# Seven products instead of eight in the first batch's last matrix product, with the folded weights split early and kept in DRAM

## What is computed

```python
def _moe_ref(x, domain_probs, w1, w2):          # x (1536, 512), w1 (4, 512, 1024), w2 (4, 1024, 512)
    p = domain_probs / (domain_probs.sum(-1, keepdims=True) + 1e-09)
    for e in range(E):
        h = np.maximum(x @ w1[e], 0.0)
        out += p[:, e:e + 1] * (h @ w2[e])

def _moe2_ref(x, w1, w2, w3, w_out):            # w1, w2 (512, 1024), w3 (1024, 1024), w_out (1024, 512)
    a = x @ w1
    b = x @ w2
    h = a * b @ w3
    return h @ w_out
```

## Time and profile before

| | |
|---|---|
| median of 3 runs | 793.29 us (792.9 to 794.73) |
| time of the profiled execution | 793.14 us |
| its span, first to last instruction | 791.3 us |
| mean granted TensorE clock | 0.998 |
| busy in the span: PE, POOL, DVE, ACT | 785.2, 537.3, 480.8, 340.1 us |
| gated layer of the first batch on PE | to 429.81 us |
| last product of the first batch on PE | 429.81 to 464.60 us |

### The profile page before, as it was taken

The page is one execution under the profiler, slowest core; times in us unless marked ns, Lnnn a source line. Parts: engine busy times, 40 slices in busy tenths (PEclk is TensorE's granted clock), DMA queues, the critical chain, the costliest instruction groups (busy, mean ns, idle before and its releaser), DMA issues.

```text
span 791.3 us, 14038 instructions
## 1 busy us (share of the span) xinstructions
PE 785.2 (99%) x4702; PEld 747.4 (94%) x4702; DVE 480.8 (61%) x1045; ACT 340.1 (43%) x731; POOL 537.3 (68%) x501
## 2 busy tenths in 40 slices
PE   9999999999999999999999999999999999999997
PEld 8777779999999999999999899999999999999997
DVE  6896687513533633624866438458568569688771
ACT  5576785432431521522444337317327327333341
POOL 3589898694683765658497427938938848944772
PEclk9999999999999999999999999999999999999999
DMA  7943565965564544636199723472472581568512
GB/s 249 401 167 113 196 223 199 369 237 196 200 238 155 213 173 186 219 150 237 72 342 378 286 65 116 126 270 104 145 274 81 154 288 64 155 204 307 182 27 85
DMA packets 53628, 155.19 MB, mean 196 GB/s; under 512 B 6176, under 2 KB 12336, under 8 KB 53552
## 3 DMA queue, kind: packets, MB, share of 16 engines
q1 hardware_dynamic: 50176, 147.24, 51.9%
q10 hardware_dynamic: 3312, 6.95, 2.5%
q0 software_dynamic: 64, 0.03, 0.1%
HBM read 103.31 MB, written 50.88 MB: 195 GB/s over the span
## 4 chain that ended last, share of the span: by engine, by line
PE 98%; POOL 1%; ACT 0%; DVE 0%; issue 0%; ACTq 0%
PE bank L50 30%; PE bank L52 30%; PE bank L51 30%; PE bank L627 3%; PE bank L637 3%; PE bank L656 3%; PE bank L243 1%; POOL pr L513 1%; PE bank L257 0%; ACT pr L520 0%; POOL bl L1354 0%; ACT pt L537 0%; DVE end L2387 0%; DVE rden L589 0%; DVE blank L2811 0%
## 5 line engine op out<-in xcount | busy, mean ns | idle before, releaser
L50 PE MATMUL bank<-bh,ah 128*128 128x384 f32 x672 | 225.3, 335 | 0.1
L52 PE MATMUL bank<-bh,al 128*128 128x384 f32 x672 | 224.6, 334 | 0.0
L51 PE MATMUL bank<-bl,ah 128*128 128x384 f32 x672 | 224.5, 334 | 0.0
L50 PEld LDWEIGHTS bank<-bh,ah 128*128 128x128 f32 x672 | 126.2, 188 | 1.4 <-issue 0.7
L51 PEld LDWEIGHTS bank<-bl,ah 128*128 128x128 f32 x672 | 126.2, 188 | 0.1
L52 PEld LDWEIGHTS bank<-bh,al 128*128 128x128 f32 x672 | 126.2, 188 | 0.0
L50 PE MATMUL bank<-sh,ah 128*128 128x384 f32 x280 | 93.8, 335 | 0.0
L52 PE MATMUL bank<-sh,al 128*128 128x384 f32 x280 | 93.6, 334 | 0.0
L51 PE MATMUL bank<-sl,ah 128*128 128x384 f32 x280 | 93.6, 334 | 0.0
L1295 POOL TENSOR_TENSOR al<-raw,ah 128x512 fp32r<-128x512 f32 (+1 forms) x60 | 71.9, 1215 | 26.7 <-ACT ah L1289 26.7
L50 PE MATMUL bank<-hh,w2h 128*128 128x384 f32 x256 | 85.5, 334 | 0.0
(11 more groups left out here) (183 smaller groups left out, 1628.1 us busy)
## 6 DMA issues: line engine op xcount, KB each, us to landing
raw<-weights SPq DMA_DIRECT2D x56, 512.0 KB, 3.5
splits<-ah SPq DMA_DIRECT2D x24, 896.0 KB, 4.1
splits<-al SPq DMA_DIRECT2D x24, 896.0 KB, 6.3
ah<-splits SPq DMA_DIRECT2D x48, 256.0 KB, 3.5
al<-splits SPq DMA_DIRECT2D x48, 256.0 KB, 4.3
ah<-splits SPq DMA_DIRECT2D x24, 384.0 KB, 4.7
al<-splits SPq DMA_DIRECT2D x24, 384.0 KB, 5.7
k<-k SPq DMA_DIRECT2D x8, 704.0 KB, 6.8
```

What stands on the lines that cost most here:

```text
L50: nc.tensor.matmul(out, wh, xh, start=start, stop=False, skip_group_check=adds_on)
L51: nc.tensor.matmul(out, wh, xl, start=False, stop=False, skip_group_check=adds_on)
L52: return nc.tensor.matmul(out, wl, xh, start=False, stop=stop, skip_group_check=adds_on)
```

## The change

The first batch's last product is made by channels with seven products too. For that the gated groups of the first batch make the sums T1 to T4 over pairs as the second batch does (`gated_group`, `pair_sum`), and DVE also takes the low parts of T1 and T2 (`pair_split_low`); POOL takes those of T3, T4 and B11 behind the weight splits. The folded weights come as four pieces `("fold", e)`, one in each expert of the first batch, are split like a group's weights, stored, and loaded for both batches (`load_last`); their splitting at the end of the second batch goes away. The raw slots and half of the gate tile serve as room for sums and outputs in between, so `down_sums` of the second batch's second down piece comes later. In both last products the second half (d = 1) has another order of products, `LAST_ORDER`. The output is by channels for both batches. The diff, cut to its core:

```diff
+LAST_ORDER = (1, 2, 6, 5, 7, 4, 3)
...
-            order += [("up", g + 4), ("up", g + 5), ("up", g + 6)]
+            order += [("fold", e), ("up", g + 4), ("up", g + 5), ("up", g + 6)]
         order += [("up", g) for g in range(19, UPS)]
-        order += [("last", j) for j in range(4)]
-        order += [("down", n) for n in range(2 * DOWNS * (E + 1))]
+        order += [("down", n) for n in range(2 * DOWNS * E)]
...
+    def stores(self, sp, t, d, *places):
+
+        for p, done in enumerate(((11, 22), (21,), (12,))):
+            for r in places:
+                self.load_split(sp, r, p)
+            for c in done:
+                self.store_end(sp, t, d, c)
...
         j += 1
+        if self.batch_of(stage) is not None:
+            self.down_group(pe, j, 1, (0, 1))
+            self.down_group(pe, j, 6, (0, 1))
+            self.down_group(pe, j, 1, (2, 3))
+            self.down_group(pe, j, 5, (0, 1))
+            self.down_group(pe, j, 2)
+            self.down_group(pe, j, 6, (2, 3))
+            self.down_group(pe, j, 5, (2, 3))
+            for p in (7, 4, 3):
+                self.down_group(pe, j, p)
+            return
...
-        pe.wait_ge(self.drained, 8 * E)
-        self.y_step(pe, t, 0, 0)
...
-        for r in range(3, ROWS_OUT):
-            for k in range(KF):
-                self.y_step(pe, t, r, k)
+        self.down_groups(pe, (E + 1) * t, i0 + KF - 1)
...
             if q == 1:
-                self.pair_high(act, p, T1)
-            self.gated_kept(act, q)
...
+                self.pair_high(act, t, p, T1)
+            self.gated_kept(act, t, q)
+            if t == 0 and q < KF - 3:
+                self.up_high(act, self.ring(i0 + q + 3))
             if q % 2 == 0:
                 if p:
-                    self.pair_high(act, p - 1, T3)
...
+                    self.pair_high(act, t, p - 1, T3)
+                    self.pair_high(act, t, p, T1)
+            elif q < KF - 1:
+                self.gated_h22(act, t, p)
+                self.pair_high(act, t, p, T2)
+                self.pair_high(act, t, p, T4)
...
         self.sums_low(pool, i0 + 1, T1, T2, T3)
+        if e == 0:
+            self.down_sums(pool, 1)
         self.parts_low(pool, e, 2, 5)
...
+    def first_gated_gpsimd(self, pool):
+
+        on, r = self.nc.gpsimd, self.ring(KH * E + 3)
+        self.up_sums(pool, r)
+        self.b_split_low(pool, on, B22, 1)
+        self.up_low(pool, r)
+        for n in range(1, KF - 3):
+            self.up_sums(pool, r + n)
+            self.up_low(pool, r + n)
+        for p in range(KH - 1):
+            self.gated_h11_low(pool, 0, p)
+        for p in range(KH):
+            self.pair_lows(pool, 0, p, T3)
+            if p == KH - 2:
+                self.gated_h11_low(pool, 0, p + 1)
+            self.pair_lows(pool, 0, p, T4)
+        for b in (B11, B21, T1, T2, B22):
+            self.b_split_low(pool, on, b, 2)
+        self.down_sums(pool, 0)
...
+    def pair_split_low(self, dve, p, b):
+
+        dve.wait_ge(self.t_high, self.pair_count(0, p, b))
+        self.nc.vector.tensor_tensor(self.sl[b][p][:, :], self.pair_raw(0, p, b), self.sh[b][p][:, :].bitcast(F32),
+                                     ALU.subtract).then_inc(self.t4_low, 1)
+
+    def gated_group(self, dve, t, q):
+        p = q // 2
 
         def rest():
             if q and q % 2 == 0:
-                self.pair_h_low(dve, p - 1, 22)
-                self.pair_sum(dve, p - 1, T3)
+                self.pair_h_low(dve, t, p - 1, 22)
+                self.pair_sum(dve, t, p - 1, T3)
             if q == 1:
-                self.pair_sum(dve, p, T1)
-            if q == KF - 1:
-                self.down_s1_s3(dve, self.nc.vector, 2 * DOWNS * E + 2)
-
-        self.gated_sums(dve, 1, q, rest)
+                self.pair_sum(dve, t, p, T1)
+            elif t == 0 and q % 2:
+                self.pair_split_low(dve, p, T1)
+
+        self.gated_sums(dve, t, q, rest)
         if q % 2 == 0:
             if q:
-                self.pair_sum(dve, p, T1)
+                self.pair_sum(dve, t, p, T1)
+            if t == 0 and q:
+                self.pair_split_low(dve, p - 1, T2)
             return
```

More of the change, by code:

```diff
@@ L993, in transfers @@
         kind, n = self.pieces()[m]
-        return 4 if kind == "down" and n >= 2 * DOWNS * E else 1
+        return 4 if kind == "fold" else 1
     def wait_raw(self, eng, kind, n):
@@ L1042, in gate_load @@
     def gate_load(self, eng, n):
+        if n == E:
+            for s in range(2):
+                eng.wait_ge(self.y_stored[s], 16 * (DOWNS * len(ENDS) // 2))
         if n > E:
@@ L1174, in up_quarters, with groups_before, wait_loaded @@
-    def up_quarters(self, g):
-        raw, s = self.raw_of("up", g), self.a_sum
+    def groups_before(stage):
+        if stage == 0:
+            return UPS - KH
+        return UPS + KH * (stage - 1) + (0 if stage <= E else KF - KH)
+    def wait_loaded(self, eng, r, a):
+        p = [a in part for part in LOADS].index(True)
+        s = self.slot_at(r)
+        nth = sum(self.slot_at(q) == s and self.user(q)[0] != "down" for q in range(RING0, r + 1))
+        eng.wait_ge(self.split_loaded[s][p], 32 * nth)
@@ L2187, in gpsimd @@
-        for j in range(4):
-            self.out_low(pool, "last", j)
-        for b in (B11, B21, B22):
-            self.b_split_low(pool, on, b, 2)
-        for n in range(2):
-            self.down_sums(pool, n)
+        self.first_gated_gpsimd(pool)
         for e in range(E):
```

813 lines of the change are left out of this document (399 added, 414 removed).

## The result

The changed kernel takes 801.8 us in the median of 6 runs (798.68 to 803.45), the one before 793.73 us beside it: 0.94% slower, ratio 1.0094 with a 95% interval of 1.0071 to 1.0117. The forecast was 799.5 us, range 795.0 to 802.0. The profiled execution is the slowest of the six, 803.45 us, span 801.4; it had 0.8 us more of stops while `Fold` ran than the kernel before, ahead of anything that was changed, so it is read here for its stops and not for its total. A stop is time in which PE starts no matmul; a step (k = 0 to 3) of a product of the last product is the three matmuls for one pair of groups, and a piece of the folded weights is one quarter of them, two steps of each product. A lock is DVE and POOL holding each other up.

The account below looks back on a forecast made before the run. The prediction took TensorE (PE), busy 99% of the span, as the bound, with POOL full in two stages. Its terms: 793.14 − 3.59 − 0.4 + 5.6 + 0.6 + 1.8 + 2.4 = 799.55, forecast 799.5 us, range 795.0 to 802.0.

Parts of the forecast that it names:

- Matmuls, −3.59: First batch's last product: 168 matmuls taking 29.12 us replace 32.71 us, saving 3.59 us.
- Splits at the end, −0.4: End of the second batch: PE's stalls from splitting the folded weights go away, saving 0.4 us.
- Gated layer, +5.6: First batch's gated layer: late POOL and ACT delay product 7 by 5.2 us, T4 adds 0.4; +5.6 us.
- the six locks: First batch's gated layer: six DVE instructions with two SBUF inputs each cost POOL 0.55 us, 3.3 us together.
- T2's low of the last pair, +0.6: Start of the first batch's last product: this low delays product 6's fourth step by 0 to 1.5 us, taken as +0.6.
- Order in the second half, 2 × 0.9: Second half of both last products: product 4 directly after 7 waits for u3, 0.9 us each, +1.8 together.
- Sums of the second down piece, +2.4: Second batch's first expert: the sums on a full POOL delay T2's low for the last group; +2.4 us.
- rival 2: POOL's lead keeps gated-layer and first-expert delays from PE; only 0.6 and 1.8 us losses remain, 791.55 us; chance 0.12.
- The sign of being wrong: Second batch's first expert: POOL idling longer than 2.4 us before group 27's sums would show the prediction wrong.
- What I cost at nothing: First batch's fold pieces in its experts, and folded-part and activations' loads (0 to 0.7 us each), were given no cost.
- Rival 1: DVE and POOL get past each other: gated layer only +1.2 to +2.5 us, total 795.15 to 796.5; chance 0.20.
- rival 4: A load of second-half folded weights or activations lands late, 1 to 3 us on top, 801 to 803; chance 0.05.

Follow-up runs that it names:

- e3: Changed kernel with ACT making the pair sums' highs ahead of the later group's weights' highs in the first batch's gated layer; 797.14 us, ratio 1.0043.
- e12: Changed kernel with DVE's lows of T1 and T2, second to fourth pair, reading one input from PSUM (results not right); 799.86 us, ratio 1.0065.
- e11: Changed kernel measured once more without any edit; 800.19 us, ratio 1.0082.
- e1: Changed kernel with the second half of both last products in the old order, nine matmuls between products 7 and 4; 805.97 us, ratio 1.0143.
- e2: Changed kernel with the second down piece's four sums at the start of POOL's first expert of the second batch; 796.95 us, ratio 1.0034.
- e10: As e9, with the gate's load in the second batch's second to fourth experts issued two groups later; 790.9 us, ratio 0.9955.
- e4: Changed kernel with the second batch's activations' load issued behind the folded weights' third load instead of ahead of it; 809.99 us, ratio 1.02.
- e7: As e6, with the second half of both last products in the old order; 795.45 us, ratio 1.0018.
- e5: Changed kernel with the edits of e2 and e3 together; 795.82 us, ratio 1.0037.
- e6: As e5, with the last folded piece's S1 and S2 loaded earlier, and the second piece's S parts first in the first batch; 794.55 us, ratio 1.0004.
- e9: As e6, with a third order in both last products' second half, and the third piece's S parts first in the first batch; 792.53 us, ratio 0.9975.

## Why the prediction was right, and what in it was not

The direction, the mechanism and the place of the three large losses were right. The total is in the range partly because two errors cancel, and that part is luck. By its steps:

- **Matmuls, −3.59.** From the first matmul of the last product (434.60) to the next group (470.14) are 35.54 us; less 2.08 and the stops of 4.29 that is 29.17, forecast 29.12.
- **Splits at the end, −0.4.** Right: no stop at u2 there.
- **Gated layer, +5.6.** 3.8 measured. Mechanism right (e3, e12), the size off: the six locks are there, but they cost POOL 0.19 to 0.33 us each and 1.8 in all, not six times the 0.55 that I took for DVE's whole instruction, 3.3. That difference of 1.5 is most of the miss. I also let all of it fall due in one stop of 5.2. The trace has 0.39, 0.75 and 0.75 at three groups and 0.3 where product 1 waits for T4's sum (forecast 0.4): a stop of PE in one group gives POOL and ACT that much time before the next, so the delay is spread, and with the restarts the stops up to and with the one at 425.77 add up to 3.5.
- **T2's low of the last pair, +0.6.** 0: product 6's fourth step never waited for it, in the changed kernel as in e11.
- **Order in the second half, 2 × 0.9.** 0.93 and 0.93. But I took the order for a pure loss; e1 shows that without it the loads cost more than it does.
- **Sums of the second down piece, +2.4.** 2.5, and e2 removes them. The size was right, a step to it was not: "POOL is as full" there, with 0.37 us idle, leaves out 13.78 and 3.19 us that it waits for ACT earlier in the same expert (14.91 and 3.18 in the changed kernel). Only what stands behind those waits is full. So a lead of POOL when it enters this expert, from which rival 2 expected a rescue, could not have helped, since POOL waits for ACT there anyway. The sign of being wrong, POOL idle for over 2.4 us before group 27's sums, taken word for word, came true while the stop came too: it was a bad sign, because it matters where the idle time lies.
- **What I cost at nothing.** Wrong. Loads cost 3.4 us in the first batch's last product and 1.5 in the experts in the profiled execution, 1.5 and 1.4 in e11; 0 to 0.7 each was the bound that I gave. The step that failed is "they land in 3 to 6 us and are wanted some 6 after issue": with the folded parts' loads, group 23's stores and the activations in the same 25 us, the DMA share is 0.97 at 350 GB/s from 432 to 457 us and 1.02 at 365 GB/s from 445 to 460, the loads of low parts land in 6.5 us in the median and 7.5 at most, and the store of group 23's low parts takes 11.0 and holds back the third piece's loads. The fold pieces in the first batch's experts did cost nothing.

Added up: the layer and T2's low were 2.4 us too dear, the loads 3 to 5 too cheap. Rival 1 (the layer at +1.2 to +2.5) was 1.3 us short of the measured 3.8, the forecast 1.8 too high. Rival 4 (a load lands late, 1 to 3 us) happened together with the forecast, with 4.9 us in the profiled execution and 2.9 in e11. Rival 2 did not, but e2 and e3 show what it would have taken: once both ties are cut, u3 is covered and the loads are apart, e10 is 3.3 us under the kernel before in medians, of the 4.0 that the change takes away.

Open: why the gate's load beside the weights' parts stops PE in the second batch's experts in the changed kernel (0.5 to 1.9 us) and not in the kernel before, which issues it at the same place. e10 shows that moving it removes the stops, not why they were not there earlier. How far ahead of the gate's load the low S parts are issued does not settle it alone: issued 0.84 us ahead of it, they landed in 5.5 us in the kernel before and in 7.2 in e2. Nor was it shown why the A parts of the last piece land 2 to 3 us later in some executions of the same kernel.

## What to carry to other kernels

Where an engine that is 68% busy on the page is full in one stage, its time there is the price of all that is hung on it, and any in-order engine that waits for it (here ACT) passes the lateness on to whatever stands behind: put what the critical path needs ahead of that wait (e3, 3 us here). Work whose inputs are there early goes into the idle time of such an engine (e2, 3 us): read its waits stretch by stretch before calling it full. Before a new stream of loads is costed at nothing, add up the bytes in its stretch against the rate that the rows show; the 384 KB low parts, put at 3 to 6 us here, took 6.5 with the DMA engines full, and a store of 896 KB beside them 11.0. And count the cover of every wait that reordering uncovers (0.82 us here, five matmuls), but look at what the order does for the loads before calling it a loss.

## What was not expected of the hardware

- A stop of PE behind a late load can cost more than itself: after the stops of 2.0 to 4.6 us (e1 twice, e4 twice, e7, e10) the granted clock fell to 0.50, the 1.2 GHz level, and 9 to 17 matmuls started 0.32 us apart, 1.3 to 2.5 us more for each stop. After the stops of up to 1.9 us (e5, e6) it stayed at 1.0.
- The mutual hold between DVE and POOL is lopsided in cost: DVE's instructions of 0.56 us take 0.77 to 1.30 in the gated layer, POOL loses 0.19 to 0.33 beside each.
- A load of 384 KB that another queue issued (the gate, 144 packets) made weight parts issued beside it land in 8.3 instead of 5.3 us, though the DMA engines' share was no higher with it (0.72 in e9) than without (0.79 in e10, both from 515 to 540 us).
